# Attention and two expert layers in one kernel: new start-up order, one multiplication on the scalar engine, a second expert's weights requested earlier, empty tiles left by one branch

## What is computed

```python
# attention, q k v: (8, 8, 576, 64)
q_s = exp(q - max(q, -1)) / (sum(...) + 1e-9)          # softmax over the 64 of a head
k_s = exp(k - max(k, axis=2)) / (sum(..., axis=2) + 1e-9)  # softmax over the 576 rows
kv  = einsum('bhsd,bhse->bhde', k_s, v)
x   = einsum('bhsd,bhde->bhse', q_s, kv)               # -> (4608, 512)
# first layer, w_in (512, 2048), w_out (2048, 512)
h = x @ w_in;  g = h - tanh(h);  x = g @ w_out
# second layer: 8 experts, one per token, w1 (8, 512, 1024), w2 (8, 1024, 512)
xn, en = x / (|x| + 1e-6), emb / (|emb| + 1e-6)
logits = xn @ en.T / tau;  e = argmax(logits);  gate = softmax(logits)[e]
out[token] = gate * (relu(x @ w1[e]) @ w2[e])
```

## Time and profile before

| | us |
|---|---|
| median of 3 runs | 1462.12 |
| lowest and highest | 1461.95, 1463.83 |
| the profiled execution's own time | 1462.44 |
| its span, first to last instruction | 1460.3 |
| PE busy | 1418.1 (97%) |
| DVE busy | 910.0 (62%) |
| ACT busy | 759.6 (52%) |
| POOL busy | 393.0 (27%) |

### The profile page before, as it was taken

How to read it: one execution, slowest core, us unless ns; L and a number is a source line. 1 busy time by engine, 2 the same in 40 slices (tenths; PEclk the granted TensorE clock), 3 DMA queues, 4 the chain that set the end, 5 groups by cost and what they waited for, 6 DMA issues and landing times.

```text
span 1460.3 us, 27446 instructions
## 1 busy us (share of the span) xinstructions
PE 1418.1 (97%) x8120; PEld 1222.8 (84%) x8121; DVE 910.0 (62%) x1771; ACT 759.6 (52%) x1558; POOL 393.0 (27%) x346
## 2 busy tenths in 40 slices
PE   5999999999999999999999999999999999999996
PEld 4888888888888888888888889877888888888885
...
GB/s 213 139 107 83 2 57 40 71 50 48 2 47 34 62 50 50 24 1 71 36 61 25 23 1 80 1 101 211 122 39 93 108 38 62 134 43 43 43 34 26
DMA packets 140197, 90.36 MB, mean 62 GB/s; under 512 B 116504, under 2 KB 120856, under 8 KB 139936
## 3 DMA queue, kind: packets, MB, share of 16 engines
...
## 4 chain that ended last, share of the span: by engine, by line
PE 87%; DVE 7%; DMA 2%; issue 2%; ACT 1%; SPq 0%; ACTq 0%; DVEq 0%; POOL 0%; POOLq 0%
PE ps L543 26%; PE ps L544 25%; PE ps L545 25%; PE ps L740 2%; PE ps L621 2%; DVE gs L1027 1%; PE ps L712 1%; PE ps L643 1%; PE ps L632 1%; PE ps L627 1%; DMA w_raw<-w 1%; DMA xrow<-scratch 1%; PE ps L663 1%; DVE gs L1024 1%; PE ps L586 1%
## 5 line engine op out<-in xcount | busy, mean ns | idle before, releaser
L1431 POOL TENSOR_TENSOR g_lo<-gs,g_hi 128x384 fp32r<-128x384 f32 x192 | 197.1, 1027 | 575.7 <-ACT g_hi L836 575.7
L543 PE MATMUL ps<-x_hi,wi_hi 128*128 128x384 f32 x768 | 278.8, 363 | 2.7 <-DVE wi_lo L1161 1.1
L544 PE MATMUL ps<-x_lo,wi_hi 128*128 128x384 f32 x768 | 260.6, 339 | 0.0
L545 PE MATMUL ps<-x_hi,wi_lo 128*128 128x384 f32 x768 | 260.5, 339 | 0.0
L826 ACT ACTIVATE usq<-ps 128x384 f32<-128x384 f32 x192 | 94.2, 491 | 295.5 <-PE ps L545 295.1
L543 PE MATMUL ps<-wo_hi,g_hi 128*128 128x512 f32 x576 | 228.3, 396 | 3.6 <-POOL g_lo L1431 2.4
L544 PE MATMUL ps<-wo_lo,g_hi 128*128 128x512 f32 x576 | 229.2, 398 | 0.0
L545 PE MATMUL ps<-wo_hi,g_lo 128*128 128x512 f32 x576 | 227.6, 395 | 0.0
L943 ACT ACTIVATE hb<-ps 128x512 f32<-128x512 f32 x74 | 44.3, 598 | 302.9 <-PE ps L545 302.9
L1024 DVE SCALAR_TENSOR_TENSOR gs<-gs,ps 128x384 f32<-128x384 f32 x192 | 105.9, 552 | 149.2 <-ACT gs L831 148.8
L1027 DVE TENSOR_TENSOR gs<-gs,usq 128x384 f32<-128x384 f32 x192 | 175.8, 915 | 0.0
...
## 6 DMA issues: line engine op xcount, KB each, us to landing
w_raw<-w SPq DMA_DIRECT2D x10, 2048.0 KB, 9.2
xrow<-scratch SPq DMA_DIRECT2D x37, 257.0 KB, 2.7
k_sb<-k SPq DMA_DIRECT2D x60, 144.0 KB, 3.4
q_sb<-q SPq DMA_DIRECT2D x60, 144.0 KB, 3.2
v_sb<-v SPq DMA_DIRECT2D x60, 144.0 KB, 3.5
...
scratch<-pad_d SPq DMA_DIRECT2D x8, 257.0 KB, 4.6
```

What stands on the lines that cost most here:

```text
L543: mm(out_, a_hi, b_hi, start=first, stop=False)
L544: mm(out_, a_hi, b_lo, start=False, stop=False)
L545: return mm(out_, a_lo, b_hi, start=False, stop=last)
L1431: G.tensor_tensor(g_lo[:, (s - 1) % 3], gs[:, (s - 1) % 2], g_hi[:, (s - 1) % 3].bitcast(F32), ALU.subtract).then_inc(glo_ready, 1)
```

## The change

It touches three stretches of the program.

1. **Start-up.** The identity is the first DMA on ACT's queue and has a semaphore of its own, for which alone PE waits. ACT waits for the constants instead. The scaling of k by v in the start-up units goes from DVE to ACT (`ACT.Copy` with a scale). The embeddings' three steps are spread otherwise, and their sum of squares writes to SBUF instead of PSUM. The tables of PE, ACT, DVE and POOL are new; SP's is as it was. PSUM banks A, Bk, C become 6, 7, 5 instead of 5, 6, 7.
2. **Table.** The scratch of the table moves from w1's to w2's landing place, so w1 of the second expert can be requested while the table is being computed, on a new semaphore `second_known`. Tile 3's rows are loaded by ACT, and w2 of the second expert behind the rows of tile 4. `lo_of_first(3)` goes behind the choice of experts of the last block.
3. **Empty tiles.** On PE, ACT, DVE and POOL the branches of the tiles 36 to 42 are nested, so the first empty one leaves all. SP goes through its last waits from tile 42 down.

```diff
@@ STARTUP: first lines of the tables for PE, ACT, DVE and POOL @@
-        "kT:0 row:0 kT:1 row:1 kT:2 row:2 kT:3 row:3 qa:0 kv:0 qa:1 qb:0 kv:1 out:0 kv:2 qb:1 qa:2 kv:3 qb:2 "
+        "kT:0 row:0 kT:1 row:1 kT:2 qa:0 kT:3 qb:0 row:2 qa:1 row:3 kv:0 qb:1 kv:1 kv:2 out:0 qa:2 kv:3 out:1 "
...
-        "qexp:0 qexp:1 row:0 row:1 qa:0 qexp:2 row:2 qb:0 qexp:3 out:0 qa:1 row:3 qa:2 qb:1 wi:0 qb:2 qa:3 "
+        "row:0 qexp:0 qexp:1 qa:0 row:1 qa:1 qb:0 row:2 qexp:2 kv:0 qb:1 qexp:3 row:3 kv:1 kv:2 out:0 qa:2 "
...
-        "kT:0 qmax:0 row:0 kT:1 qmax:1 row:1 qsum:0 kT:2 qmax:2 qsum:1 kT:3 qmax:3 row:2 row:3 kv:0 qsum:2 "
-        "qsum:3 kv:1 kv:2 out:0 kv:3 out:1 wi:0 out:2 out:3 qmax:4 emb:0 kT:4 wo:0 qsum:4 row:4 chunk:0 wi:1 "
+        "kT:0 qmax:0 row:0 emb:0 qmax:1 kT:1 qsum:0 row:1 qsum:1 kT:2 qmax:2 kT:3 row:2 qmax:3 row:3 kv:0 "
+        "qsum:2 kv:1 kv:2 qsum:3 out:0 wi:0 kv:3 out:1 qmax:4 kT:4 out:2 out:3 row:4 qsum:4 wi:1 chunk:0 wo:0 "
...
-    at[0] = raw_at
+    at[0] = raw_at + 4 * DC * F2
...
-    assert at[0] <= raw_at + 4 * DC * F2
+    assert at[0] <= raw_at + 4 * DC * F2 + 4 * FC2 * D
...
-    A, Bk, C = ps[:, 5], ps[:, 6], ps[:, 7]
+    A, Bk, C = ps[:, 6], ps[:, 7], ps[:, 5]
...
+        def second_expert(load_w, ready):
+
+            with sp.If(sp.value_load(e_two[0:1, 0:1], min_val=0, max_val=1) > 0):
+                e1 = sp.value_load(e_list[0:1, 1:2], min_val=0, max_val=E - 1)
+                sp.wait_ge(w_ready, ready)
+                load_w(e1)
+
+        sp.wait_ge(second_known, 1)
+        second_expert(load_w1, 1)
         sp.wait_ge(tab_ready, 1)
         sp.wait_ge(rows_stored, 16 * GPB * NBLK)
         sp.wait_ge(pads_stored, 16 * E)
-        load_rows(KNOWN, KNOWN)
-
-        with sp.If(sp.value_load(e_two[0:1, 0:1], min_val=0, max_val=1) > 0):
-            e1 = sp.value_load(e_list[0:1, 1:2], min_val=0, max_val=E - 1)
-            sp.wait_ge(w_ready, 1)
-            load_w1(e1)
-            sp.wait_ge(w_ready, 2)
-            load_w2(e1)
+        sp.wait_ge(out_stored[0], 16)
+        load_rows(4, 0)
+        second_expert(load_w2, 2)
...
+        ahead(0)
+        for j in range(1, 4):
+            sp.wait_ge(out_stored[j], 16)
+            load_rows(4 + j, j)
+            ahead(j)
+        with sp.Fori(1, LOOPS) as i:
...
-        for t in range(SURE - 4, TILES):
+        for t in reversed(range(SURE - 4, TILES)):
...
-        pe.wait_ge(cst_in, 32)
+        pe.wait_ge(ident_in, 16)
...
+            pe.wait_ge(xlo_b, UPB + 1)
...
-        for t in range(4 * LOOPS, TILES):
-            slot(t, t % 4, t + 1 < TILES, t + 2 < TILES)
+        with contextlib.ExitStack() as while_live:
+            for t in range(4 * LOOPS, TILES):
+                while_live.enter_context(live(pe, t))
+                slot(t, t % 4, t + 1 < TILES, t + 2 < TILES)
...
+        act.dma_start(ident[:], ident_d).then_inc(ident_in, 16)
         act.dma_start(embs[:], emb).then_inc(emb_in, 16)
-        act.dma_start(ident[:], ident_d).then_inc(cst_in, 16)
+        act.dma_start(cst[:], cst_d).then_inc(cst_in, 16)
         act.dma_start(tri_f[:], tri_d).then_inc(tri_in, 16)
-        act.dma_start(cst[:], cst_d).then_inc(cst_in, 16)
         act.dma_start(rows[:], rows_d).then_inc(rows_in, 16)
         act.dma_start(rtau[:], tau.partition_broadcast(P)).then_inc(tau_in, 16)
+        act.wait_ge(cst_in, 16)
...
+            if what == "kv":
+
+                act.wait_ge(kv_step, u * 2 + 2)
+                for h in range(2):
+                    a = slice(h * HD, (h + 1) * HD)
+                    last = fn(kv_[a, a], bankA[a, 0:HD], ACT.Copy, scale=krec_[a, 1:2])
+                last.then_inc(kvb_ready, 1)
...
+        act.wait_ge(tab_ready, 1)
+        act.wait_ge(rows_stored, 16 * GPB * NBLK)
+        act.wait_ge(pads_stored, 16 * E)
+        act.dma_start(xrow[:, KNOWN], scratch[ds(entry(KNOWN, T_ROW, ROWS - P), P), :]).then_inc(row_in[KNOWN], 16)
+
         relu(2, 2, 0)
         h_split(1, 1)
         relu(2, 2, 1)
-        act.wait_ge(tab_ready, 1)
...
+                if t is None:
+                    return
...
-                dve.wait_ge(tri_in, 16)
-                V.tensor_copy(tri[:], tri_f[:]).then_inc(tri_ready, 1)
                 dve.wait_ge(emb_in, 16)
-                dve.wait_ge(xlo_b, UPB + 1)
-                V.tensor_tensor_reduce(C[0:E, 0:D], embs[:], embs[:], 1.0, 0.0,
+                junk = gs[0:E].rearrange("p i n -> p (i n)")[:, 0:D]
+                V.tensor_tensor_reduce(junk, embs[:], embs[:], 1.0, 0.0,
                                        ALU.mult, ALU.add, accum_out=ss[0:E, 0:1]).then_inc(en_ss, 1)
             elif i == 1:
                 dve.wait_ge(en_nrm, 1)
@@ -1177,12 +1204,14 @@
                 V.reciprocal(nrm[0:E, 0:1], nrm[0:E, 0:1]).then_inc(en_step, 1)
                 dve.wait_ge(en_step, 2)
                 V.tensor_scalar(embs[:], embs[:], nrm[0:E, 0:1], None, ALU.mult).then_inc(en_ss, 1)
-                dve.wait_ge(cst_in, 32)
+                dve.wait_ge(tri_in, 16)
+                V.tensor_copy(tri[:], tri_f[:]).then_inc(tri_ready, 1)
+            else:
+                dve.wait_ge(cst_in, 16)
                 V.tensor_copy(run[:], cst[:, C_BASE:C_BASE + E])
                 dve.wait_ge(rows_in, 16)
                 dve.wait_ge(tau_in, 16)
                 V.reciprocal(rtau[:], rtau[:])
-            else:
...
-        lo_of_first(3)
         for g in range(GPB):
             route_part("tail_logits", NBLK - 1, g)
         route_part("choose", NBLK - 1, 0)
+        lo_of_first(3)
         route_part("dest", NBLK - 1, 0)
...
-        V.tensor_scalar(e_two[:], before[:, E1:E], 1.5, None, ALU.is_ge)
+        V.tensor_scalar(e_two[:], before[:, E1:E], 1.5, None, ALU.is_ge).then_inc(second_known, 1)
```

More of the change, by code:

```diff
@@ L250, in both_banks @@
     def both_banks(u):
[L252 removed]
+        return (ps[:, 6:8], ps[:, 0:2], ps[:, 2:4], ps[:, 4:6])[u if u < UPB else 0]
     tail_ps = A, Bk, y_ps[1]
@@ L756, in slot @@
         def slot(t, j, ahead1, ahead2):
[L757 to L769 removed]
+            now = weights_of(t)
+            if ahead1:
+                with live(pe, t + 1):
+                    hidden(t + 1, (j + 1) % 4, 0, *weights_of(t + 1))
+            hidden_T(t, j)
+            if ahead2:
+                with live(pe, t + 2):
+                    rows_T(t + 2, (j + 2) % 4)
+            if ahead1:
+                with live(pe, t + 1):
+                    hidden(t + 1, (j + 1) % 4, 1, *weights_of(t + 1))
+            second(t, j, *now)
         rows_T(1, 1)
@@ L999, in _ @@
                 slot(i * 4 + j, j, True, True)
-        for t in range(4 * LOOPS, TILES):
-            slot(t, t % 4, t + 1 < TILES, t + 2 < TILES)
+        with contextlib.ExitStack() as while_live:
+            for t in range(4 * LOOPS, TILES):
+                while_live.enter_context(live(act, t))
+                slot(t, t % 4, t + 1 < TILES, t + 2 < TILES)
     @block.vector
@@ L1413, in _ @@
         scaled(4 * LOOPS, 0, 16 * LOOPS)
-        for t in range(4 * LOOPS + 1, TILES):
-            with live(dve, t):
+        with contextlib.ExitStack() as while_live:
+            for t in range(4 * LOOPS + 1, TILES):
+                while_live.enter_context(live(dve, t))
                 splits(t, t % 4, t + 1 < TILES, t + 2 < TILES)
@@ L1493, in _ @@
                 slot(i * 4 + j, j)
-        for t in range(4 * LOOPS, TILES):
-            slot(t, t % 4)
+        with contextlib.ExitStack() as while_live:
+            for t in range(4 * LOOPS, TILES):
+                while_live.enter_context(live(pool, t))
+                slot(t, t % 4)
     block.__exit__(None, None, None)
```

81 lines of the change are left out of this document (33 added, 48 removed), and 21 rows, old and new, of tables (ACT, DVE, PE).

## The result

| | median, us | lowest to highest | runs |
|---|---|---|---|
| before | 1462.03 | 1461.01 to 1463.83 | 4 |
| changed | 1449.34 | 1449.17 to 1449.81 | 4 |

The ratio is 0.9912, with a 95% interval of 0.9895 to 0.9930: 12.9 us less, between 10.2 and 15.4. The forecast was 1451.0. The profiled execution has 1449.26 us with a span of 1447.2, so it can be set against the 1460.3 of before: 13.05 less.

What follows compares the result with a forecast made beforehand. PE was taken as the limit from 57 us on, DVE as fullest from 33 to 57. Start-up 5.0, table 2.6 and end 3.6 less sum to 11.2; from 1462.4, and 0.3 less against the median: 1451.0 us, 8-in-10 range 1446.0 to 1456.0.

Steps and rivals of the forecast that it cites:

- A ledger of an engine's work: Start-up, DVE's work up to chunk 2: at most 4.1 us less, of which 3.0 taken for chunk 2's start.

Runs made afterwards that it cites:

- e8: The changed kernel with w1 of the second expert requested only when tile 3's rows have landed; 1455.50 us, ratio 0.9954.

## What to carry to other kernels

Before a load is moved, list everyone that waits for it, in-order engines that split or copy it included: the wait that the profile puts first may not be the one that the load's time is worth most to (e8: the rows land 2 us sooner, and the kernel is 6 slower, by the weights and what hangs on them). Price a change by the stretches of several executions; here a stretch of half clock came and went in the same place without any edit, and one pair of traces would have given its 2.7 us to whatever was nearby. A ledger of an engine's work up to a point tells when that work is done (3.4 us earlier here, 3.0 foreseen), but not which of it the next product waits for: look that operation up, and where it now stands.

## What the runs showed of the chip

- Beside a 2 MB load on SP's queue a transfer of 257 KB on another queue, a load from ACT or a store from POOL, took 4.3 to 5.1 us when it was requested 4 to 5 us behind the load; a store took 7.0 to 8.2 when 1.3 behind it. Alone both took 2.6 to 2.9, but for single ones of up to 4.3. The Trainium skill (DMA: Bandwidth & Descriptors, Queues, rings and completion order) has the DMA engines take turns between queues packet by packet. By that rule the time should not depend on how much of the load is left; the stores of 7 to 8 us, which landed within 1.6 us of the load, go against it, and the rows and stores of 4.3 to 5.1 would fit either.
- The granted clock was half for 3.4 or 6.8 us on end inside the program, behind places where PE had waited or behind the small products of the logits near 980 us, in some executions and not in others with the same code in that place.
- A branch on ACT was followed by 4.0 to 4.7 us of nothing while weights were loading, in eight of the fourteen kernels.
- The drain that ends POOL's program takes 3.1 us without the nesting and 3.8 with it, and ended 4.3 us after the start of the last store's issue in the changed kernel. What the nesting does is to start it earlier.
